# Attention and two MLPs on one core: segment sums of the first band in PSUM, and a new order of the first stage

## The reference

```python
def _attn_ref(q, k, v):                       # q, k, v: (4, 8, 576, 64)
    q_d, k_d, v_d = (means of 4 neighbouring rows of q, k, v)      # 144 rows
    out_d = softmax(q_d @ k_d.T / 8) @ v_d
    out_up = np.repeat(out_d, 4, axis=2)
    mask = np.abs(pos[:, None] - pos[None, :]) < 4                 # a band of 7
    out_local = softmax(where(mask, q @ k.T / 8, -1e9)) @ v
    return out_up + out_local
x = attn.transpose(0, 2, 1, 3).reshape(2304, 512)
x = np.maximum(x @ w_in, 0) ** 2 @ w_out                           # d_ff 2048
return maximum(maximum(x @ w1, x @ w2), x @ w3) @ w_out2           # d_ff 768
```

## Time and profile before

| what | value |
|---|---|
| median of 3 runs | 937.86 us (933.24 to 944.39) |
| the profiled execution | 944.06 us |
| its span, first to last instruction | 942.3 us |
| TensorE matmul busy | 840.0 us (89%) |
| VectorE busy | 513.9 us (55%) |
| ScalarE busy | 324.6 us (34%) |
| GpSimd busy | 226.7 us (24%) |
| mean granted TensorE clock | 0.936 |

### The profile page before, as it was taken

The page is one execution under the profiler, slowest core; times in us unless marked ns, Lnnn a source line. Parts: engine busy times, 40 slices in busy tenths (PEclk is TensorE's granted clock), DMA queues, the critical chain, the costliest instruction groups (busy, mean ns, idle before and its releaser), DMA issues.

```text
span 942.3 us, 13126 instructions
## 1 busy us (share of the span) xinstructions
PE 840.0 (89%) x5454; PEld 795.2 (84%) x5454; DVE 513.9 (55%) x505; ACT 324.6 (34%) x827; POOL 226.7 (24%) x187
## 2 busy tenths in 40 slices
PE   5934698998798899999897999989999999999995
PEld 4524697898797799898797999989999999999994
DVE  6499965689977488896499400672122221222111
ACT  3344345443445435463435353322121212111111
POOL 0188942123231133431145232310000000000000
PEclk9556989999899999999899899999999999999998
DMA  9910214001341010520010001622011111100001
GB/s 218 348 33 1 59 41 99 18 1 25 85 111 26 2 35 21 140 61 14 29 27 1 23 2 43 199 90 90 1 34 34 34 34 33 35 20 15 9 26 33
DMA packets 40011, 50.62 MB, mean 54 GB/s; under 512 B 9744, under 2 KB 30224, under 8 KB 39056
## 3 DMA queue, kind: packets, MB, share of 16 engines
q1 hardware_dynamic: 38644, 49.19, 18.8%
q10 hardware_dynamic: 1308, 0.59, 0.3%
HBM read 38.27 MB, written 11.50 MB: 53 GB/s over the span
## 4 chain that ended last, share of the span: by engine, by line
PE 66%; DVE 16%; ACT 6%; POOL 5%; DMA 3%; issue 3%; SPq 1%; ACTq 0%; DVEq 0%
PE PS L430 19%; PE PS L432 19%; PE PS L431 19%; DVE qk L857 3%; DVE tmp L846 3%; PE PS L473 2%; DVE tmp L793 2%; DVE sc L804 2%; DMA v_tok<-v 2%; PE PS L493 2%; PE PS L465 1%; PE PS L521 1%; ACT qkT L632 1%; POOL G L1048 1%; POOL WI L1033 1%
## 5 line engine op out<-in xcount | busy, mean ns | idle before, releaser
L430 PE MATMUL PS<-XS,WI 128*128 128x384 f32 (+2 forms) x768 | 244.7, 319 | 2.5 <-DVE XS L990 2.5
L431 PE MATMUL PS<-XS,WI 128*128 128x384 f32 (+2 forms) x768 | 241.0, 314 | 0.0
L432 PE MATMUL PS<-XS,WI 128*128 128x384 f32 (+2 forms) x768 | 241.0, 314 | 0.0
L1048 POOL TENSOR_TENSOR G<-g,G 128x256 fp32r<-128x256 f32 (+1 forms) x128 | 135.3, 1058 | 329.8 <-ACT G L684 329.8
L430 PE MATMUL PS<-G,WO 128*128 128x256 f32 (+1 forms) x512 | 160.6, 314 | 10.7 <-POOL G L1048 10.4
L431 PE MATMUL PS<-G,WO 128*128 128x256 f32 (+1 forms) x512 | 155.4, 304 | 0.0
L432 PE MATMUL PS<-G,WO 128*128 128x256 f32 (+1 forms) x512 | 155.3, 303 | 0.0
L430 PEld LDWEIGHTS PS<-XS,WI 128*128 128x128 f32 x768 | 147.7, 192 | 7.8 <-issue 3.5
L431 PEld LDWEIGHTS PS<-XS,WI 128*128 128x128 f32 x768 | 147.6, 192 | 1.5
L432 PEld LDWEIGHTS PS<-XS,WI 128*128 128x128 f32 x768 | 147.4, 192 | 0.0
L430 PEld LDWEIGHTS PS<-G,WO 128*128 128x128 f32 x512 | 101.5, 198 | 13.0 <-POOL G L1048 11.8
(11 more groups left out here) (93 smaller groups left out, 1201.4 us busy)
## 6 DMA issues: line engine op xcount, KB each, us to landing
...
```

The lines of the kernel that those rows point to most:

```text
L430: mm(dst, wt(HI), xt_(HI), start=first, stop=False)
L431: mm(dst, wt(HI), xt_(LO), start=False, stop=False)
L432: return mm(dst, wt(LO), xt_(HI), start=False, stop=last)
L1048: Q.tensor_tensor(G[:, s % NGR, LO, :cnt], g32[:, s % 2, :cnt], G[:, s % NGR, HI, :cnt].bitcast(f32), ALU.subtract).then_inc(g_ready, 1)
```

## The change

All chunks and segments are 18 rows, or 288 tokens, wide. `qk` tasks take 3 sums of rows, "x" tasks 6 rows (three per chunk). In batch 0, segment 0 keeps its scores and its accumulator in PSUM banks 3 to 5, which nothing else uses until the first `down`; only the last addition writes to `qk`. v is summed by four additions of GpSimd. VectorE splits no weight tiles: GpSimd makes all 32, 14 of them ahead of the first "x" parts, 4 behind these, and two behind each of the first seven blocks. The pooled output of batch 0 is scaled on ScalarE two heads at a time (`norm_pair`, `scale_pair`) and moved from SBUF to SBUF by 16 DMAs (`move_pair`) instead of through DRAM; `add_pooled(0)` stands behind the first two score steps of segment 1. The later batches have two buffers for products instead of one. The tasks have new places, an "o" comes one group later, a first segment's Exp stands ahead of an "s" task (`EXP_BEFORE`), and `read_x2` stands behind place 1.

```diff
...
+HR = GL // 2
+CR = [HR * n for n in range(2 * NB + 1)]
+NCH = len(CR) - 1
...
+CH = NG * HR
+BATCH = [CR[n] // GL for n in range(NCH)]
+ROWS = [(CR[n] - GL * BATCH[n], CR[n + 1] - GL * BATCH[n]) for n in range(NCH)]
...
-    parts = [(j0, min(j0 + POOL, NJ)) for j0 in range(0, NJ, POOL)]
+    parts = [(j0, j0 + 3) for j0 in range(0, NJ, 3)]
...
+XP = [(m, m + 3) for m in range(0, HR, 3)]
+X = [("x", t) for t in range(len(XP))]
+X0 = X[:len(X) // 2]
...
-for n in range(NH + 3):
-    heads.append(([("o", n - 3)] if n >= 3 else []) + ([("s", n)] if n < NH else []))
+for n in range(NH + 4):
+    heads.append(([("o", n - 4)] if n >= 4 else []) + ([("s", n)] if n < NH else []))
     heads.append([("t", n - 2)] if 2 <= n < NH + 2 else [])
-VSUM = [("v", 0), ("v", 1)]
-first_tasks = qk_tasks(0) + heads0[:2] + VSUM + heads0[2:] + X[:2]
+first_tasks = qk_tasks(0) + heads0 + X0
...
-QK_AT = {1: (1, 0, 3), 2: (2, 10, 0), 3: (4, 9, 1)}
-HEADS_AT = {1: (1, 2, 2), 2: (2, 11, 0), 3: (4, 11, 0)}
-STRIDE = {1: 3, 2: 4, 3: 4}
-X_AT = {0: [None, None, (0, 13, 1), (0, 14, 1), (0, 15, 1)],
-        1: [(1, 14, 1), (1, 15, 1), (1, 15, 3), (2, 5, 1), (2, 6, 1)],
-        2: [(3, 13, 1), (3, 14, 1), (3, 15, 1), (4, 4, 1), (4, 5, 1)],
-        3: [(5, 13, 1), (5, 14, 1), (5, 15, 1), (6, 8, 1), (6, 9, 1)]}
-EXP_AT = {(0, 4): 1, (1, 6): 2, (1, 15): 3, (2, 15): 4, (3, 14): 5, (4, 15): 6, (5, 12): 7}
+QK_AT = {1: (1, 0, 3), 2: (2, 13, 0), 3: (4, 12, 0)}
+HEADS_AT = {1: (1, 2, 2), 2: (2, 14, 2), 3: (4, 13, 2)}
+STRIDE = {1: 2, 2: 3, 3: 3}
+X_AT = {0: [None, None, None, (0, 13, 1), (0, 14, 1), (0, 15, 1)],
+        1: [(1, 13, 1), (1, 14, 1), (1, 15, 1), (2, 7, 1), (2, 8, 1), (2, 9, 1)],
+        2: [(3, 13, 1), (3, 14, 1), (3, 15, 1), (4, 7, 1), (4, 8, 1), (4, 9, 1)],
+        3: [(5, 13, 1), (5, 14, 1), (5, 15, 1), (6, 8, 1), (6, 9, 1), (6, 10, 1)]}
+EXP_BEFORE = {1: 1, 2: 6, 3: 6}
+EXP_AT = {(0, 4): 1, (2, 1): 3, (3, 15): 5, (5, 15): 7}
...
-ATT = (6, 7, 0, 1, 2, 3)
+ATT = (6, 7, 0, 1, 2)
...
-        return (4, 5, 0, 2, 1, 3)[at] if b == 0 else at % 2
-    if kind == "v":
-        return 4 + task[1]
+        return (4, 3, 2, 1, 0, 4)[at] if b == 0 else at % 2
     if kind == "x":
...
+        return (1, 0, 4)[task[1]] if b == 0 and task in X0 else 1 - task[1] % 2
...
-W_BY_DVE = 4
-W_AHEAD = 20
+W_AHEAD, W_BEFORE_X = 18, 14
...
+    first_acc = PS[:, 3:6, :].rearrange("p b c -> p (b c)")
+    def scores_of(n):
+        return first_acc[:, HR * D:HR * (D + BAND)].rearrange("p (i o) -> p i o", o=BAND) if n == 0 else sc[:]
+    def acc_of(n):
+        lo, hi = ROWS[n]
+        return first_acc[:, :HR * D].rearrange("p (i d) -> p i d", d=D) if n == 0 else qk[:, lo:hi, :]
     def k_rows(lo, hi):
...
+    def move_pair(e, pair, n):
+        e.wait_ge(pair_scaled, pair + 1)
+        for h in (2 * pair, 2 * pair + 1):
+            e.dma_start(odg[n * P // 2 + h:(n + 1) * P // 2:NH], od_st[:, 2 * h + n, :D]).then_inc(pair_moved, 16)
...
+        for pair in range(NH // 2):
+            move_pair(sp, pair, 0)
+            if pair < NH // 2 - 1:
+                move_pair(sp, pair, 1)
...
-            filled(sp, b - 1, X[2])
+            filled(sp, b - 1, X0[-1])
             load_q(b, 0)
...
-            filled(sp, b - 1, X[4])
+            filled(sp, b - 1, X[-1])
...
-                        for t in VSUM:
-                            read(pe, b, t)
+                        pe.wait_ge(vd_made, 2)
...
-                for n_ in (4, 5):
-                    pe.wait_ge(att_free[n_], uses[n_])
+                pe.wait_ge(att_free[4], uses[4])
+                pe.wait_ge(band_out, 1)
...
-        def pooled_out_store():
-            act.wait_ge(od_scaled, 1)
-            act.dma_start(od_dram[0].rearrange("h (n p) d -> p (h n) d", n=2),
-                          od_st[:, :, :D]).then_inc(od_stored, 16)
-        def pooled_out_load():
-            act.wait_ge(od_stored, 16)
-            act.dma_start(view(odg[:], "p j d -> p (j d)"), od_dram[0].rearrange("h (g j) d -> g h (j d)", j=NJ)).then_inc(od_loaded, 16)
-        w = [W_BY_DVE]
+        def scale_pair(pair):
+            act.wait_ge(pair_normed, pair + 1)
+            rec = view(hst[:], "p h n -> p (h n)")
+            for c in range(4 * pair, 4 * pair + 4):
+                last = A(od_st[:, c, :D], od_st[:, c, :D], ACT.Copy, scale=rec[:, c:c + 1])
+            last.then_inc(pair_scaled, 1)
...
+            if task == ("s", 1):
                 band_probs(0)
             attend(0, task)
-            if task[0] == "o" and task[1] < NH - 1:
-                split_next(1)
-        split_next(2)
-        pooled_out_store()
-        split_next(3)
-        pooled_out_load()
+            if task[0] == "o":
+                h = task[1]
+                if h in (3, 5, 6):
+                    scale_pair((h - 2) // 2)
+                if h < 6:
+                    split_next(2)
+        scale_pair(NH // 2 - 1)
+        move_pair(act, NH // 2 - 1, 1)
         split_next(W_AHEAD)
-        attend(0, X[0])
-        attend(0, X[1])
+        for task in X0:
+            attend(0, task)
+        def woven(s, place):
+            for b, task in PLAN.get((s, place), []):
+                if task == ("s", EXP_BEFORE.get(b)):
+                    band_probs(FIRST[b])
+                attend(b, task)
         for s in range(TOTAL):
             n, f = divmod(s, NF)
-            for b, task in PLAN.get((s, 0), []):
-                attend(b, task)
+            woven(s, 0)
             square(s)
-            if f == 1 and n:
-                read_x2(n - 1)
             for i in w_late(s):
...
-            for place in range(1, PLACES):
-                for b, task in PLAN.get((s, place), []):
-                    attend(b, task)
+            woven(s, 1)
+            if f == 1 and n:
+                read_x2(n - 1)
+            woven(s, 2)
+            woven(s, 3)
...
-                made["acc", o] = count(V.tensor_tensor(acc, acc, own[o % m], ALU.add))
+                to = acc if o < BAND - 1 else qk[:, lo:hi, :]
+                made["acc", o] = count(V.tensor_tensor(to, acc, own[o % m], ALU.add))
...
-            dve.wait_ge(od_loaded, 16 * (b + 1))
-            acc = view(qk[:, lo:hi, :], "p (j t) d -> p j t d", t=POOL)
-            add = odg[:, lo // POOL:hi // POOL, :].unsqueeze(2).broadcast_to([P, (hi - lo) // POOL, POOL, D])
+            if b:
+                dve.wait_ge(od_loaded, 16 * b)
+            else:
+                dve.wait_ge(pair_moved, 16 * 2 * NH)
+            j0, j1 = -(-lo // POOL), hi // POOL
+            if lo < POOL * j0:
+                acc = qk[:, lo:POOL * j0, :]
+                link(V.tensor_tensor(acc, acc, odg[:, j0 - 1:j0, :].broadcast_to([P, POOL * j0 - lo, D]), ALU.add))
+            if hi > POOL * j1:
+                acc = qk[:, POOL * j1:hi, :]
+                link(V.tensor_tensor(acc, acc, odg[:, j1:j1 + 1, :].broadcast_to([P, hi - POOL * j1, D]), ALU.add))
+            acc = view(qk[:, POOL * j0:POOL * j1, :], "p (j t) d -> p j t d", t=POOL)
+            add = odg[:, j0:j1, :].unsqueeze(2).broadcast_to([P, j1 - j0, POOL, D])
             V.tensor_tensor(acc, acc, add, ALU.add).then_inc(band_out, 1)
             dve.wait_ge(band_out, n + 1)
...
-        def split_w(i):
-            w_landed(dve, i)
-            link(V.tensor_copy(w_tile(i, HI), w_raw(i)))
-            V.tensor_tensor(w_tile(i, LO), w_raw(i), w_tile(i, HI).bitcast(f32), ALU.subtract).then_inc(w_ready_dve, 1)
+        def norm_pair(pair):
+            read(dve, 0, ("o", 2 * pair + 1))
+            rec = view(hst[:, 2 * pair:2 * pair + 2, :], "p h n -> p (h n)")
+            link(V.tensor_scalar(rec, od_st[:, 4 * pair:4 * pair + 4, D], EPS, float(POOL), ALU.add, ALU.mult))
+            V.reciprocal(rec, rec).then_inc(pair_normed, 1)
...
+        two = [tmp[:, 0], tmp[:, 1]]
+        three = two + [early[:, 0]]
...
-        seg = score_steps(0, bufs(0, True))
-        run(seg, 5)
+        seg = score_steps(0, three)
+        run(seg, 6)
         head_max(0, 0)
+        run(seg)
+        softmax_in(0)
+        head_max(0, 1)
+        softmax_out(0)
+        head_max(0, 2)
+        dve.wait_ge(v_loaded, 48)
+        seg = value_steps(0, three)
+        for h in range(3, NH):
+            run(seg, 1)
+            head_max(0, h)
+            if h >= 5 and h % 2:
+                norm_pair((h - 5) // 2)
         run(seg, 1)
-        head_max(0, 1)
+        norm_pair(2)
         run(seg)
-        head_max(0, 2)
-        softmax_in(0)
-        head_max(0, 3)
-        softmax_out(0)
-        head_max(0, 4)
-        dve.wait_ge(v_loaded, 48)
-        seg = value_steps(0, bufs(0, True))
-        run(seg, 1)
-        for h in range(5, NH):
-            head_max(0, h)
-            run(seg, 1)
-        run(seg, 1)
-        scale_pooled(0)
-        run(seg)
-        for i in range(W_BY_DVE):
-            split_w(i)
-        add_pooled(0)
+        norm_pair(3)
         dve.wait_ge(q_loaded[1], 16)
         dve.wait_ge(k_loaded, 32)
```

(64 more changed lines are left out.)

146 lines of the change are left out of this document (60 added, 86 removed).

## The result

The changed kernel took 912.67 us (median of four, 910.28 to 913.78) against 936.76 us of the kernel before on the same chip (four, 933.24 to 944.39): ratio 0.973, 95% interval 0.966 to 0.979. The forecast of 933 is 20 us too high; 911 was the number of rival 1. The profiled execution took 910.28 us, its span is 908.5 us and the mean granted clock 0.955.

The account below looks back on a forecast made before the run. TensorE's waits at the start, then GpSimd, later TensorE broken by waits and low clock, bound the kernel. -10.6 at the first border + 5.4 later = -5.2 us: 944.06 becomes 938.9 profiled, median 933; range 912 to 948.

Parts of the forecast that it names:

- rival 1: Later chunks: the new TensorE waits don't come, as VectorE and loads are in time; -27 us, 911; chance 0.33.
- Chunks of 288: All chunks: a matmul pitch of 0.1333 us leaves the 3072 matmuls at 409.6 us; chunk 0 takes 5.1 us more.
- Ahead of the first `up`: Kernel start: VectorE's additions end at 62.8 us and the first `up` starts at 69.2, 14 us earlier.
- The wait at 2.7 behind Exp 3: Chunk 2, block 7: the x task is due at 29.8 us, TensorE there at 24; +7.5 us with clock.
- the signs by which I would have called the forecast wrong: Waits at chunk 2's block 7 and chunk 4's block 12 missing, or chunk 1 starting after 146 us.
- What GpSimd takes back: Chunk 0: three blocks at 3.3 us, then 6.65 each; chunk 1 at 140, leaving 10.6 of 14 us.
- rival 3: Kernel start: PSUM operations cost as next to GpSimd, first `up` later; about 0 gain, 938; chance 0.07.
- the later chunks' sum: Chunk 1 onward: waits gained and lost, -4 - 8 - 10 + 7.5 + 14.5 + 7 - 1.6 = +5.4 us.
- Chunk 1 and the entry to chunk 2: Earlier q and k sums -4, fewer "o" waits -8, shorter waits into chunk 2 -10 us.
- The -8 for "o" tasks: Chunk 1: "o" tasks, a group later, lose most of 10.3 us of waits and some low clock; -8 us.
- into chunks 4 and 6: Chunk borders: segment 4 added 2 us late, Exps 5 and 7 hold ScalarE; chunk 4 +7, chunk 6 -1.6 us.
- 2.13 and 4.12: Chunk 2 block 13, chunk 4 block 12: waits of 3.7 and 6.9 us for pooled q and k; +14.5 us.

Follow-up runs that it names:

- run 3: The changed kernel with segment 0's scores and accumulator in SBUF again, not PSUM: 922.64 us, ratio 0.982.
- run 8: The changed kernel with VectorE splitting the first four weight tiles again, ahead of segment 1's scores: 915.65 us, ratio 0.972.
- run 5: The changed kernel with v summed by TensorE again, GpSimd's four additions taken out: 912.12 us, ratio 0.974.
- run 6: The changed kernel with batch 0's pooled output through DRAM in two transfers instead of 16 moves: 912.08 us, ratio 0.974.
- run 4: The changed kernel with Exp 3 moved back behind block 15 of chunk 1, from block 1 of chunk 2: 903.84 us, ratio 0.963.
- run 9: The changed kernel with Exp 1 behind `square` 2 of chunk 0, not `square` 4: 915.31 us, ratio 0.972.
- run 1: The changed kernel with the heads' old, wider strides in batches 1 to 3 (3, 4, 4 places): 912.5 us, ratio 0.9715.
- run 7: The changed kernel with one product buffer, not two, in batches 1 to 3: 914.12 us, ratio 0.977.
- run 10: The changed kernel with the heads' old strides and one product buffer in batches 1 to 3 together: 921.28 us, ratio 0.977.

## Why the prediction was wrong

**Right.** *Chunks of 288*: matmuls start 0.13 us apart, and the second stage is unchanged. *Ahead of the first `up`*: 14 us earlier forecast, 15.1 measured; vd at 30.5 (31), additions ended at 61.2 (62.8), first `up` at 68.1 (69.2). The way there is shown by runs 3, 8, 5 and 6, each undone by itself: 10.5 + 3.0 + 1.0 + 0.2 = 14.7 us, nearly the whole, if they add up, which no run shows. The price of 1.27 us for an operation with its accumulator in PSUM was right: 1.35 in its row, 1.26 to 1.27 from one start to the next. Here the Trainium skill, "SBUF — State Buffer", Who interferes with whom, agrees with the trace: 1.35 beside 1.26 us with one SBUF input, 2.3 to 2.4 on both sides with two (run 3). The Trainium skill's rule against small transfers, from "DMA: Bandwidth & Descriptors", Rules for kernel authors, agrees with the trace for the single transfer: a move of 18 KB took 3.1 to 3.4 us to land, the pooled load of 288 KB 3.5. But the last moves did not pay it one behind the other, as I feared (VectorE found odg complete at 58.59), and the time does not tell the 16 moves from the round trip through DRAM: 912.7 and 912.1 us. No run makes the moves one transfer.

**Right in place, and near in size.** The wait at 2.7 behind Exp 3: 5.55 us; run 4 prices it at 6.4 (profiles) to 9 (medians) with its clock, +7.5 forecast. The wait at 4.12 came too, smaller than forecast: 4.64 us. Both had their stretch of half clock, and chunk 1 did not start after 146, so that none of the signs by which I would have called the forecast wrong showed, and its time was wrong all the same. Half of rival 1's reason ("the new waits don't come") did not hold either; that its 911 came out is in part luck.

**Failed: "What GpSimd takes back".** Chunk 1 was put at 140 and started at 134.7. I had three blocks undisturbed and let GpSimd eat 3.4 us of the start (the 14 us less 5.1 of width would have given 136.6). There were four, and the whole start came through: runs 3 and 8 shift the first `up` and chunk 1 by the same amount (10.5 and 10.5, 3.0 and 3.0). The reason that fits is that Exp 1 stands at a block and so moves with the `up`: its place in blocks does change the border (run 9: 3.7 us for two blocks). Of the 28.6 us between forecast (938.9) and profiled run (910.28), 5.3 are at this border, and GpSimd's rows hold 4.6 of them: block 0's G ended at 76.05 and not 78.4 (the x parts 1.5 earlier, four splits in 6.1 us and not 6.9), and block 7's at 110.0 and not 114.6, by the fourth undisturbed block. It also prices rival 3 wrongly: without PSUM the kernel loses 10 us, none of which "GpSimd would have lost anyway".

**Failed: the later chunks' sum.** Forecast +5.4 apart from width; measured, against the first profile of the kernel before, from chunk 1 to the end 773.8 us for 796.8, -17.9 without the width. That is the other 23.3 us. Against its second profile it is -15.1, or -15.7 up to the second stage, and by stretch:

- Chunk 1 and the entry to chunk 2: forecast -22, measured -6.5, a miss the other way. The waits of 2.41, 3.68 and 7.13 us went as forecast, but for 1.19. The -8 for "o" tasks was put here and stood elsewhere: of their 10.3 us only 0.9 were in chunk 1 before (4.3 in chunks 2 and 3, 5.0 in 4 and 5). In the changed kernel it is 4.7 here, 0.7 and 1.6. The 4.7 go with the denser heads (run 1 has 0.5 in all).
- Chunks 2 and 3: forecast about +19 (7.5, some 5 of the 14.5, and 7 ahead of chunk 4), measured +1.2. The 5.55 us came; the wait at 2.13 was 1.8 us and not 3.7. What did not come is the wait ahead of chunk 4, 1.38 us (1.09 before).
- Chunks 4 and 5: forecast about +8, measured -5.0. One wait of 4.64 us came, where 6.9 was forecast. The wait ahead of chunk 6, which counts here, fell from 3.60 to 1.38 us, and some low clock behind smaller waits went.
- Chunks 6 and 7: forecast nothing, measured -5.4. In chunk 6 TensorE waits 0.44 us where it waited 2.1 (1.1 in the second profile), the 6.8 us of half clock at its start are gone, and the wait ahead of the second stage is 2.23 us (2.50 before, 3.56 in the second profile).

Two steps failed here. The first is "into chunks 4 and 6", +7 and -1.6: I took VectorE to be 2 us late for segment 4's x task, from the heads' last minimum. It was 2.9 us early (the addition, from 340.31, ended at 342.0, wanted at 344.91), and both borders wait 1.38 us. The denser heads and the second buffer each make part of the room. Without the first (run 1) the waits ahead of chunks 4 and 6 are 3.89 and 3.09 us, without the second (run 7) 3.09 and 1.37, without both (run 10) 3.50 and 5.87, with 3.59 for segment 4's x task. I had written that the second buffer "saves some 0.1 us an operation" and counted the strides by places alone; together with the clock they are 10.4 us.

The second is the size of "2.13 and 4.12", the largest term: forecast +14.5. Its waits are 9.9 us (1.8, 4.6 and, ahead of "s" 0, 2.2 and 1.3) and 6.8 us of half clock, some 13 against 8.4, so about +5. I had taken 16 us from the last x task to the pooled transposes; they were 14.2 and 13.8 (257.80 to 272.00, 387.19 to 401.03). At 4.12 some 2 us of that are q's load, 4.7 us from its issue (387.71) to VectorE's sum, where the kernel before took 6.7 (issued at 400.87, the sum at 407.53); why it was shorter, no run shows.

**Open.** Run 10 gives back 10.4 of some 15 us. Of the remaining 5 some may be chance (the two profiles of the kernel before differ by 2.9 us from chunk 1 to the end); the rest must lie in what was not undone by itself: `read_x2` behind the q and k sums, the Exps ahead of "s" tasks, chunks of equal width. No run separates these.
